# MLP steps of a three-stage kernel on one core: a sum moved ahead of a range reduction, a copy moved to the front of each step, and weight sums moved from GpSimd to VectorE

## What is computed

```python
def _moe_ref(x, domain_probs, w1, w2):            # 1536 x 512, E = 4, F = 1024
    p = domain_probs / (domain_probs.sum(-1, keepdims=True) + 1e-09)
    for e in range(E):
        h = np.maximum(x @ w1[e], 0.0)
        out += p[:, e:e + 1] * (h @ w2[e])

def _moe2_ref(x, w_in, w_out):                    # d_ff = 2048
    h = x @ w_in
    g = h * np.cos(h)
    return (g @ w_out).astype(np.float32)
```

## Time and profile before

| | before |
|---|---|
| median of 3 runs | 849.49 us (847.65 to 849.9) |
| profiled execution, its own time | 849.18 us |
| span of the profiled execution | 847.3 us |
| PE busy | 807.1 us, 95% |
| DVE busy | 640.8 us, 76% |
| ACT busy | 346.4 us, 41% |
| POOL busy | 339.8 us, 40% |

### The profile page before, as it was taken

One profiled execution on the slowest core, in us unless ns is written; L12 is line 12 of the kernel. 1 busy time (PEld: TensorE's weight loads), 2 busy tenths in 40 slices (PEclk: granted clock), 3 DMA queues, 4 the chain that ended last, 5 costly groups with the idle time before them and its releaser, 6 DMA issues.

```text
span 847.3 us, 12076 instructions
## 1 busy us (share of the span) xinstructions
PE 807.1 (95%) x4501; PEld 683.6 (81%) x4501; DVE 640.8 (76%) x1013; ACT 346.4 (41%) x706; POOL 339.8 (40%) x332
## 2 busy tenths in 40 slices
PE   8999999999999999999999999858998898988998
PEld 7888888888888888888888888737887787877876
DVE  7987766676676676676676676996988878898876
ACT  4643232222222222222222223467666666565663
POOL 4975343333333333334324324763433324243221
PEclk9999999999999999999999999988999999999999
DMA  9832110111111110110110111000001100000003
GB/s 332 322 122 62 38 38 26 59 54 37 26 38 38 63 48 27 38 39 26 38 38 26 38 38 37 8 31 26 26 25 38 39 26 25 26 26 25 2 1 149
DMA packets 19869, 44.86 MB, mean 53 GB/s; under 512 B 2344, under 2 KB 2392, under 8 KB 19812
## 3 DMA queue, kind: packets, MB, share of 16 engines
q1 hardware_dynamic: 19812, 44.10, 16.1%
HBM read 40.93 MB, written 3.17 MB: 52 GB/s over the span
## 4 chain that ended last, share of the span: by engine, by line
PE 82%; DVE 11%; issue 3%; ACT 2%; DMA 1%; POOL 1%; SPq 0%; DVEq 0%; ACTq 0%
PE ps L1238 42%; PE ps L1219 36%; DVE temps L1023 3%; DVE x_sum L897 1%; PE ps L1184 1%; PE ps L1134 1%; DVE temps L1026 1%; DMA att<-att_in 1%; DVE x_lo L903 1%; DVE temps L1034 1%; ACT temps L694 1%; DVE temps L1087 1%; DVE w_lo L824 1%; DVE temps L1106 1%; PE ps L1148 1%
## 5 line engine op out<-in xcount | busy, mean ns | idle before, releaser
L488 POOL TENSOR_TENSOR h_lo<-temps,h_hi 128x512 fp32r<-128x512 f32 (+1 forms) x192 | 205.2, 1070 | 476.4 <-ACT h_hi L587 295.9
L1219 PE MATMUL ps<-x_hi,w_hi 128*128 128x512 f32 (+1 forms) x672 | 231.1, 344 | 32.0 <-DVE temps L1106 23.5
L1219 PE MATMUL ps<-x_lo,w_hi 128*128 128x512 f32 (+1 forms) x672 | 229.0, 341 | 0.0
L1219 PE MATMUL ps<-x_hi,w_lo 128*128 128x512 f32 (+1 forms) x672 | 229.0, 341 | 0.0
L1238 PE MATMUL ps<-h_hi,w_hi 128*128 128x512 f32 x576 | 228.3, 396 | 0.3 <-POOL h_lo L488 0.2
L1238 PE MATMUL ps<-h_lo,w_hi 128*128 128x512 f32 x576 | 227.4, 395 | 0.0
L877 DVE TENSOR_TENSOR y<-ps,y 128x512 f32<-128x512 f32 x252 | 172.9, 687 | 71.7 <-PE ps L1238 71.4
L1238 PE MATMUL ps<-h_hi,w_lo 128*128 128x512 f32 x576 | 225.9, 392 | 0.0
L587 ACT ACTIVATE h_hi<-temps 128x512 fp32r<-128x512 f32 (+1 forms) x128 | 67.3, 526 | 337.2 <-DVE temps L915 337.2
L1219 PEld LDWEIGHTS ps<-x_hi,w_hi 128*128 128x128 f32 x672 | 130.1, 194 | 57.2 <-DVE temps L1106 26.7
L1219 PEld LDWEIGHTS ps<-x_lo,w_hi 128*128 128x128 f32 x672 | 130.5, 194 | 17.7
(11 more groups left out here) (83 smaller groups left out, 754.6 us busy)
## 6 DMA issues: line engine op xcount, KB each, us to landing
w_raw<-w_in SPq DMA_DIRECT2D x96, 256.0 KB, 2.7
att<-att_in SPq DMA_DIRECT2D x24, 512.0 KB, 6.7
temps<-p_scr SPq DMA_DIRECT2D x4, 768.0 KB, 4.1
out<-y SPq DMA_DIRECT2D x12, 256.0 KB, 2.0
att<-dp_in SPq DMA_DIRECT2D x1, 24.0 KB
p_scr<-att SPq DMA_DIRECT2D x1, 24.0 KB
lam<-lam_in SPq DMA_DIRECT2D x1, 6.0 KB, 1.7
```

The lines of the kernel that those rows point to most:

```text
L488: pool.tensor_tensor(hs_lo[side][:, f, at], ring(s, i), f32(hs_hi[side][:, f, at]), ALU.subtract).then_inc(s_hlo, 1)
L1219: mm = pe.matmul(ps[:, bank, 0:CTS[side]], ww[q % 2][:, of], xx[side][:, 2 * x + k, :], start=(opens and k == 0 and n == 0), stop=(k == 1 ...
```

## The change

It changes orders, one engine assignment, and the waits that follow from them:

- **DVE, each MLP step:** L1106 (C12) goes ahead of less_turns(s, 2); the weights' low piece that stood before less_turns(s, 2) now follows it.
- **ACT, each MLP step:** before_p6(s) goes ahead of sine(s - 1, 2) and gate_high(s - 1, 1), which stood at the end of the step before; sine(s - 1, 3) goes behind take_u2(s).
- **Weights' sums in the MLP (quarters 17 to 23):** from POOL's queue in the wide step to DVE's in the narrow step; in the wide step the low part of piece 0 comes ahead of evict(s, 1), in the narrow step the low part of the sums comes behind gate(s - 1, 3).
- **Step 32:** T2's low part is made by DVE (x2_t_low(0, 1)); POOL's lows of the second block wait for the ninth high part and for three of DVE's lows; ACT makes x2_high(., 4) last of its side; w2_piece(q, 1) of DVE is later; P2 of step 33 gets a wait of its own.

```diff
@@ POOL
-                pool.wait_ge(s_x2hi, 9 * side + (6 if d >= KT else d + 1))
+                pool.wait_ge(s_x2hi, 9 * side + (9 if d >= KT else d + 1))
+                if d >= KT and side == 0:
+                    pool.wait_ge(s_x2lo1, 3)
...
-                    x2_t2_low(0)
-                    x2_t2_low(1)
...
-                if side == 0 and 0 < q < ALL_QUARTERS - 1:
+                if side == 0 and 0 < q < QUARTERS:
                     w_sums(q + 1)
@@ ACT
-                sine(s - 1, 3)
+                sine(s - 1, 2)
+                gate_high(s - 1, 1)
                 take_u2(s)
                 if s == STEPS:
-                    x2_high(1, 4)
                     x2_t_high(1, 0)
+                    x2_t_high(1, 1)
+                sine(s - 1, 3)
                 gate_high(s - 1, 2)
...
                 turns(s, 3)
-                sine(s, 2)
                 if more and side == 1:
                     w2_piece(q + 1, 1)
-                gate_high(s, 1)
@@ DVE
+            def w_sums(q):
...
+                dve.tensor_tensor(w_sum[:, 0, :], a21, a22, ALU.add).then_inc(s_wsum, 1)
+                dve.tensor_tensor(w_sum[:, 2, :], a11, a21, ALU.subtract).then_inc(s_wsum, 1)
+                dve.wait_ge(s_wsum, 4 * q + 1)
+                dve.tensor_tensor(w_sum[:, 1, :], w_sum[:, 0, :], a11, ALU.subtract).then_inc(s_wsum, 1)
+                dve.wait_ge(s_wsum, 4 * q + 3)
+                dve.tensor_tensor(w_sum[:, 3, :], a12, w_sum[:, 1, :], ALU.subtract).then_inc(s_wsum, 1)
...
                     x2_sum(0, 3)
+                    x2_t_low(0, 1)
                     evict(s, 0)
-                    w2_piece(q, 1)
...
                     gate(s - 1, 2)
-                    if many:
-                        evict(s, 1)
                     if more and side == 0:
                         w1_piece(q + 1, 0)
                     elif more:
+                        w_sums(q + 1)
+                    if many:
+                        evict(s, 1)
+                    gate(s - 1, 3)
+                    if more and side == 1:
                         w1_piece(q + 1, 2)
-                    gate(s - 1, 3)
                     evict(s, 2 if many else 1)
...
                 if many:
                     evict(s, 5)
+                dve.wait_ge(s_prod, product_count(s, P3))
+                dve.wait_ge(s_hlo, 4 * s + 3 - R_RING + 1)
+                dve.tensor_tensor(ring(s, 3), bank_c, u2[:, 0:CTS[side]], ALU.add).then_inc(s_c, 1)
+                less_turns(s, 2)
+                if s == STEPS:
+                    w1_piece(q + 1, 0)
                 if more and side == 0:
                     w1_piece(q + 1, 1)
                 elif more:
                     w2_piece(q + 1, 0)
-                less_turns(s, 2)
-                dve.wait_ge(s_prod, product_count(s, P3))
-                dve.wait_ge(s_hlo, 4 * s + 3 - R_RING + 1)
-                dve.tensor_tensor(ring(s, 3), bank_c, u2[:, 0:CTS[side]], ALU.add).then_inc(s_c, 1)
@@ PE
                     if i == P6:
                         pe.wait_ge(s_pre, s - STEPS + 1)
-                        if s == STEPS:
-                            pe.wait_ge(s_x2lo, 8)
-                        elif first:
-                            pe.wait_ge(s_x2lo1, 5)
+                        if first:
+                            pe.wait_ge(s_x2lo1, 4 * side + 2)
+                    if i == P2 and s == STEPS + 1:
+                        pe.wait_ge(s_x2lo, 10)
```

More of the change, by code:

```diff
@@ L722, in _ @@
                 if s == STEPS:
-                    x2_high(0, 4)
                     x2_t_high(0, 1)
@@ L742, in _ @@
                 if s == STEPS:
-                    x2_t_high(1, 1)
                     x2_t_high(1, 2)
                     x2_t_high(1, 3)
+                    x2_high(1, 4)
                 gate_high(s - 1, 3)
@@ L757, in _ @@
                 turns(s, 3)
-                sine(s, 2)
                 if more and side == 1:
                     w2_piece(q + 1, 1)
-                gate_high(s, 1)
-            sine(ALL_STEPS - 1, 3)
-            gate_high(ALL_STEPS - 1, 2)
-            gate_high(ALL_STEPS - 1, 3)
+            last = ALL_STEPS - 1
+            sine(last, 2)
+            gate_high(last, 1)
+            sine(last, 3)
+            gate_high(last, 2)
+            gate_high(last, 3)
         @block.vector
@@ L894, in x2_sum @@
                     dve.wait_ge(s_x2t, 4 * side + 2)
-                    dve.wait_ge(s_x2lo1, 3 * side + 1)
+                    dve.wait_ge(s_x2lo1, 4 * side + 1)
                     a, b = y_half(side, 0, 1), t2
@@ L899, in x2_t_low @@
             def x2_t_low(side, i):
-                dve.wait_ge(s_x2hi, (9 * side + 6 + i) if side == 1 or i else 5)
-                if side == 1 and i == 1:
+                dve.wait_ge(s_x2hi, 9 * side + 5 + i)
+                if i == 1:
                     dve.wait_ge(s_x2t, 4 * side + 4)
@@ L1035, in gate @@
                                          in1=ring(s, i), op0=ALU.subtract, op1=ALU.mult).then_inc(s_gate, 1)
+            def w_sums(q):
+                a11, a12 = w_raw[:, 0, 0:FF2], w_raw[:, 0, FF2:512]
+                a21, a22 = w_raw[:, 1, 0:FF2], w_raw[:, 1, FF2:512]
+                dve.wait_ge(s_raw[0], 16 * (q + 1))
+                dve.wait_ge(s_raw[1], 16 * (q + 1))
+                dve.wait_ge(s_whi, w1_count(q - 1))
+                dve.wait_ge(s_wlo, w1_count(q - 1))
+                dve.tensor_tensor(w_sum[:, 0, :], a21, a22, ALU.add).then_inc(s_wsum, 1)
[4 more added lines that the diff above has]
+                dve.tensor_tensor(w_sum[:, 3, :], a12, w_sum[:, 1, :], ALU.subtract).then_inc(s_wsum, 1)
             def evict(s, k):
@@ L1061, in _ @@
                     x2_sum(1, 1)
+                    x2_t_low(1, 0)
                     x2_sum(1, 2)
-                    x2_t_low(1, 0)
                     x2_sum(1, 3)
+                    x2_t_low(1, 1)
                 else:
@@ L1070, in _ @@
                         dve.wait_ge(s_x2hi, 18)
-                        dve.wait_ge(s_x2lo, 14)
+                        dve.wait_ge(s_x2lo, 12)
                     evict(s, 0)
                     gate(s - 1, 2)
-                    if many:
-                        evict(s, 1)
                     if more and side == 0:
@@ L1088, in _ @@
                 if s == STEPS:
-                    x2_t_low(1, 1)
                     x2_t_low(1, 2)
                     x2_t_low(1, 3)
-                    w1_piece(q + 1, 0)
+                    w2_piece(q, 1)
                 else:
@@ L1294, in _ @@
                         if s == STEPS + 1:
-                            pe.wait_ge(s_x2lo, 14)
+                            pe.wait_ge(s_x2lo, 8)
                     if i == P5:
@@ L1311, in _ @@
                         if first:
-                            pe.wait_ge(s_x2lo1, 2 if s == STEPS else 6)
+                            pe.wait_ge(s_x2lo1, 4 * side + 3)
                     if i == P4:
@@ L1315, in _ @@
                         if first:
-                            pe.wait_ge(s_x2lo1, 3 if s == STEPS else 7)
+                            pe.wait_ge(s_x2lo1, 4 * side + 4)
                     if i == P3:
                         pe.wait_ge(s_c, 2 * (s - STEPS) + 1)
+                        if first:
+                            pe.wait_ge(s_x2lo, 6 * (side + 1))
                     product(s, i)
```

9 lines of the change are left out of this document (2 added, 7 removed).

## The result

The changed kernel takes 836.62 us (median of 3 runs, 836.58 to 836.77) against 849.49; the ratio is 0.9854, 95% interval 0.9832 to 0.9877. The forecast was 832, the range 821 to 842. The profiled execution took 836.77 us with a span of 834.5, so the span is 12.8 us shorter.

A forecast was written before the change was run, and what follows sets the result against it. PE was taken as bound, its pairs losing 4.9 us to C12's late sum and the slow clock behind it. -12.0 - 3.8 - 0.4 - 1.5 = -17.7 us from 849.18 gave 831.5, forecast 832, range 821 to 842.

The forecast's parts named there:

- The pairs: Steps 36 to 45: C12's waits go, smaller gaps come at P4 and P3; loss 4.9 to 2.5 us, -12.0 over five.
- Slack of the downs: In the pairs: users of ACT's later sines, including PE's downs some 4 us later, were said to have slack.
- P1's copy first: ACT's copy ahead of the sines in the pairs: worth 0, bounds -0.5 and +0.5 us a pair.
- Steps 32 to 34: P5 of step 34 at about 581.4 instead of 585.18: -3.8 us, bounds 0 and -8.
- Ends: Step 35's 0.42 us of waiting goes, -0.4; steps 46 and 47 lose 1.27 and 0.3, -1.5.
- opening bound of 40 us: Whole kernel: PE busy 807.1 of 847.3 us, so at most 40 us can go with the matmuls unchanged.
- The clock falls all the same: Rival: P4 and P3 gaps make 3 us, slow clock follows, pairs gain nothing; 844 us, chance 0.14.
- PE nearly dense: Rival: h_lows miss DVE's two-input instructions, pairs lose 0.3 instead of 4.9 us; 821 us, chance 0.13.
- The reorder frees nothing: Rival: P3 or the ring's place, not the queue, holds L1106; 845 us at best, counted with the clock rival.
- the slower one: Rival: an h_low holds w_sums, L1087 ends 4 us beyond the estimate or later; 853 us, chance 0.05.
- The Trainium skill's rule: Two-SBUF-input VectorE and SBUF-reading GpSimd instructions lock each other out entirely; sums 2.5 to 2.9, pairs' gain 8 to 10 us.

The follow-up runs named there:

- copy_alone: The kernel before with only ACT's order of the change (P1's copy first, sines and gate_high later): 852.4 us, ratio 1.0037.
- c12_alone: The kernel before with only L1106 (C12) moved ahead of less_turns(s, 2) and the weights' low piece in each MLP step: 837.2 us, ratio 0.9865.
- short_lows_33: sums_in_wide_step with two weights' low parts between C22 of steps 32 and 33 made for 8 columns only (partly wrong weights): 826.5 us, ratio 0.9735.
- sums_in_wide_step: The changed kernel with the sums of quarters 18 to 23 on VectorE in the wide step, quarter 17's on POOL in step 32: 828.0 us, ratio 0.9749.
- two_sums_more: The changed kernel with two more 128x256 instructions in each w_sums on VectorE, written to overwritten places: 842.4 us, ratio 0.9913.
- sums_alone: The kernel before with only the weights' sums of quarters 17 to 23 moved to VectorE in the narrow step: 842.9 us, ratio 0.9923.
- sums_on_pool: The changed kernel with the sums of quarters 17 to 23 back in POOL's queue at the wide step: 833.4 us, ratio 0.9818.

## Why the prediction was right, and where it was not

**The pairs: right, step by step.** C12's wait goes; what was behind it in VectorE's queue comes in front of C22, whose end was put at 29.4 to 30.3 us after the wide P1 for a deadline of 27.7. In the kernel after, P3 starts 683.76 - 653.50 = 30.3 us after P1. A pair was to lose 2.5 us beyond PE's 31.2 instead of 4.9: 33.7, measured 33.83. The terms: the sums 1.6 to 2.5 with the lock, measured 677.98 - 675.54 = 2.44; the wait of 2.47 us for their high part gone; no slow clock behind waits of up to 1.2 us; P4 first, then P3. The forecast for five pairs was -12.0 us, measured -11.0. The 4.9 us that a pair lost were rightly split: 3.06 of waiting, and some 1.8 of slow clock, for which copy_alone gives 1.5 and c12_alone 1.0 (34.9 - 33.9, where P3's wait of 0.2 us goes for it).

**Slack of the downs: wrong, small.** I had given the downs' users some 4 us. The kernel after has 0.15 us of waiting there, and it is the next bound: 1.36 us with the sums on POOL.

**P1's copy first: right in the pairs of the whole change, wrong by itself.** In the whole change it takes P6's wait of 1.00 us away and the pair stays at 33.83, since C22 comes late anyway. By itself it costs 1.1 us a pair or more with the clock alike, and 3.5 us in all; the bound was 0.5.

**Steps 32 to 34: the term that failed.** It was -3.8 us and is nothing: P5 of step 34 at 585.12, before 585.18. C12 of step 32 came as forecast: I had P5 of step 33 near 567, it starts at 566.15. The error lies in step 33. P5 of step 34 was put at 581.4, so P1 of step 34 at 578.6, and that comes at 581.53. For step 33 I had charged only a gap of some 3 us at P4. It is 4.62 us, P3 waits 0.83 more, and the clock is at 1.2 GHz from 577.60 to 583.24. What I left out is VectorE's work in that step. The kernel after has four stretches by an h_low there, 1.0 to 1.1 us each over 0.68, 0.68, 0.42 and 0.42 (its timeline of VectorE, steps 32 and 33):

```profile
567.34 1.76 DVE L820 TENSOR_TENSOR w_lo<-w_raw,w_hi 128x512 fp32r<-128x512 f32 x1
...
571.28 1.78 DVE L1030 SCALAR_TENSOR_TENSOR temps<-temps 128x512 f32<-128x512 f32 x1
...
574.10 1.37 DVE L1045 TENSOR_TENSOR w_sum<-w_raw,w_sum 128x256 f32<-128x256 f32 x1
...
578.18 1.51 DVE L1022 SCALAR_TENSOR_TENSOR temps<-temps 128x256 f32<-128x256 int32 x1
```

In the kernel before VectorE had one such stretch there (1.64 us for L1026 at 568.58), and it stood idle for 3.54 us, into which two of POOL's h_lows fell (573.27 and 576.18):

```profile
577.08 1.47 DVE L824 TENSOR_TENSOR w_lo<-w_sum,w_hi 128x1024 fp32r<-128x1024 f32 x1 [3.54 <-ACT w_hi L521]
```

In the kernel after 0.7 us of idle time is left between C22 of step 32 and C22 of step 33: the stretches and the four sums have filled the rest, and C22 of step 33 starts at 579.62, against 579.86 before. I had argued from a wait (C12 comes 4 us earlier) where the step's length is VectorE's work; short_lows_33 shows that less of this work shortens it. That the four stretches can't be laid beside evictions, since step 33 has none, is argued from the order, not tried.

**Ends.** -1.5 was forecast and the last two steps gave 1.7; the 0.42 us of step 35 stayed, 0.56.

**The sum.** -17.7 us were forecast and -12.8 came (in spans): 11.0 for 12.0, nothing for 3.8 and for 0.4, 1.7 for 1.5. The time is 4.6 us above the forecast, and most of that is the term of steps 32 to 34. That the total fell well inside the range owes nothing to terms that cancel: all but one were too large. The opening bound of 40 us was loosely read: PE's busy time holds the slow clock too, and fell by 5.4 us with the same matmuls.

**The rivals.** None took place. "The clock falls all the same" failed since two waits of 0.7 and 1.2 us a pair stay at 2.4 GHz. "PE nearly dense" needs the sums elsewhere: sums_in_wide_step comes near its pair (32.0 us against 31.5), but not to its 821 us, since steps 32 to 35 give nothing there either. "The reorder frees nothing" is refuted by c12_alone. For the slower one, two_sums_more gives the price: 0.4 us a pair for each instruction, so the 4 us that it needed would have been ten more of them.

**The Trainium skill's rule** (SBUF — State Buffer, "Who interferes with whom") made the sums dearer by one wait for an h_low. The rows of L1045 (1.40 and 1.37 us) and the gate moved ahead of the eviction (1.78 us) agree with it: what is lost is the rest of POOL's instruction, not a share. In the kernel after the sums took 2.44 us, near the upper value, yet the pairs gained more than the 8 to 10 us that I had worked out with it. In sums_alone the four of step 39 took 0.41 to 0.42 us each, and the gate behind them 1.28: whichever two-input instruction starts beside the h_low pays.

## What to carry to other kernels

When an instruction moves ahead in a queue, take the next deadline on the same queue and add up the chain to it: here 3 us of waiting became 2 us at later products, and the gain was the difference plus the slow clock. Work that changes engines should go where the receiving engine waits: the same four sums on VectorE cost about 1% in the narrow step over the wide step's idle time. In step 33, where VectorE was full nearly from end to end, an earlier release gained nothing; less work on VectorE did.

## What the runs showed of the hardware that I had not expected

- A VectorE instruction with two SBUF inputs that started while a GpSimd subtraction ran ended when that did, plus 0.55 us where it had 512 columns and 0.28 where it had 256: the gate of 0.68 us took 1.78 us started 0.25 us into h_low, 1.20 started later. One with a PSUM input kept its 0.68 us. The other way round POOL's h_low, 1.27 us alone, is longer where it starts while such a VectorE instruction still runs: 1.73 us at 566.82 in the kernel after, where L1022 had 0.6 us to go.
- In steps 37 to 45 PE's clock stayed at 2.4 GHz behind waits of 0.7 and 1.2 us. The longer waits show no fixed limit: it fell to 1.2 GHz, for 9 to 19 matmuls, behind three of five waits of 1.9 us (sums_alone), one of five of 2.05 (c12_alone), five of five of 3.06 before (in two of them 0.8 and 1.6 us later) and four of five of 3.05 (copy_alone). In step 33, where waits of 1.47 and 0.97 us follow close on others, it was down as well (granted 0.50 from 566.1 to 573.0 in the kernel after).
- A PE wait that the profile calls "issue" was a wait for POOL's h_low: it ended 0.1 us after it in two kernels (h_low to 678.70 and PE from 678.80 in sums_on_pool, 677.78 and 677.88 in the kernel after).
